# Attention and two gated MLPs on one core: three loads of weights asked for tile by tile, at other places of the pairs, one of them four pairs later

## The reference

```python
mask = q_bucket[:, :, :, None] == k_bucket[:, :, None, :]
scores = scale * np.matmul(q, k.transpose(0, 1, 3, 2))
scores = np.where(mask, scores, -1000000000.0)
attn = softmax(scores)                      # with 1e-9 added to the sum
x = np.matmul(attn, v)                      # heads side by side: (1536, 512)
h = x @ moe_w_in;   g = np.where(h > 0, h, np.exp(np.minimum(h, 0)) - 1);   x = g @ moe_w_out
h = x @ moe2_w_in;  r = np.maximum(h, 0);   g = s * r * r + b;              out = g @ moe2_w_out
```

## Time and profile before

| what | value |
|---|---|
| median of three executions | 738.39 us (738.21 to 739.23) |
| the profiled execution | 738.77 us, its span 736.9 us |
| granted TensorE clock | 0.999 |
| TensorE busy | 728.1 us, 99% of the span |
| VectorE, ScalarE, GpSimd busy | 75%, 68%, 67% |
| attention | up to about 223 us |
| loads of input weights, output weights | 96 and 32 tiles of 256 KB |

### The profile page before, as it was taken

The page is one execution under the profiler, slowest core; times in us unless marked ns, Lnnn a source line. Parts: engine busy times, 40 slices in busy tenths (PEclk is TensorE's granted clock), DMA queues, the critical chain, the costliest instruction groups (busy, mean ns, idle before and its releaser), DMA issues.

```text
span 736.9 us, 14171 instructions
## 1 busy us (share of the span) xinstructions
PE 728.1 (99%) x4617; PEld 666.1 (90%) x4617; DVE 556.4 (75%) x1185; ACT 501.6 (68%) x941; POOL 496.5 (67%) x436
## 2 busy tenths in 40 slices
PE   8999999999999999999999999999999999999998
PEld 5999999999999889988998899989998999899986
DVE  6888888888888887877666777677767776766764
ACT  7888888888885767575657666577566656474552
POOL 6678899999998687835654577677655454644340
PEclk9999999999999999999999999999999999999999
DMA  5686765665524222321112223132112211131101
GB/s 167 160 177 134 162 169 138 156 170 123 136 61 107 86 89 85 115 58 58 31 56 59 61 88 110 58 95 85 52 57 78 78 47 58 58 102 43 58 1 57
DMA packets 78287, 67.82 MB, mean 92 GB/s; under 512 B 9284, under 2 KB 66964, under 8 KB 78228
## 3 DMA queue, kind: packets, MB, share of 16 engines
q1 hardware_dynamic: 77940, 66.80, 33.6%
q10 hardware_dynamic: 288, 0.26, 0.1%
HBM read 46.23 MB, written 3.19 MB: 67 GB/s over the span
## 4 chain that ended last, share of the span: by engine, by line
PE 79%; POOL 9%; DMA 4%; issue 4%; ACT 2%; DVE 2%; SPq 0%; POOLq 0%; DVEq 0%; ACTq 0%
PE acc L939 35%; PE h_ps L919 32%; PE pt_ps L859 4%; PE pv_ps L874 2%; PE pv_ps L875 2%; PE s_ps L845 2%; PE s_ps L846 2%; POOL pt_lo L562 2%; DMA x_parts<-x_second 2%; POOL qqk L550 1%; POOL pt_hi L560 1%; DMA qqk<-qqk 1%; POOL x L578 1%; POOL x_sum L569 1%; DMA qqk<-bits 1%
## 5 line engine op out<-in xcount | busy, mean ns | idle before, releaser
L624 POOL TENSOR_TENSOR wi_lo<-w_raw,wi_hi 128x512 fp32r<-128x512 f32 x96 | 98.8, 1030 | 188.6 <-ACT wi_hi L1035 186.0
L919 PE MATMUL h_ps<-xb_hi,wi_hi 128*128 128x256 f32 x672 | 190.2, 283 | 0.5 <-DVE u_sb L1362 0.5
L919 PE MATMUL h_ps<-xb_hi,wi_lo 128*128 128x256 f32 x672 | 190.2, 283 | 0.0
L919 PE MATMUL h_ps<-xb_lo,wi_hi 128*128 128x256 f32 x672 | 190.2, 283 | 0.0
L919 PEld LDWEIGHTS h_ps<-xb_hi,wi_hi 128*128 128x128 f32 x672 | 128.8, 192 | 2.6 <-DVE u_sb L1362 0.7
L919 PEld LDWEIGHTS h_ps<-xb_lo,wi_hi 128*128 128x128 f32 x672 | 128.8, 192 | 1.8
L919 PEld LDWEIGHTS h_ps<-xb_hi,wi_lo 128*128 128x128 f32 x672 | 128.8, 192 | 0.0
L629 POOL TENSOR_TENSOR wi_lo<-wi_sum,wi_hi 128x512 fp32r<-128x512 f32 x96 | 122.6, 1298 | 1.9 <-ACT wi_hi L1035 1.9
L1157 ACT ACTIVATE r_sb<-h_sb 128x512 f32<-128x512 f32 x96 | 60.0, 625 | 76.8 <-DVE h_sb L1379 76.8
L1217 DVE TENSOR_SCALAR_CACHE_REDUCE probs<-s_ps 128x768 f32<-128x768 f32 x96 | 91.8, 957 | 10.4 <-PE s_ps L846 7.6
L939 PE MATMUL acc<-g_hi,wo_late 128*128 128x512 f32 x288 | 91.8, 390 | 0.0
(11 more groups left out here) (122 smaller groups left out, 1676.1 us busy)
## 6 DMA issues: line engine op xcount, KB each, us to landing
w_raw<-w_in_dram SPq DMA_DIRECT2D x96, 256.0 KB, 3.1
wo_raw<-w_out_dram SPq DMA_DIRECT2D x32, 256.0 KB, 2.9
raw<-qk_dram SPq DMA_DIRECT2D x15, 384.0 KB, 5.8
qqk<-kt SPq DMA_DIRECT2D x15, 384.0 KB, 4.6
raw_v<-v_dram SPq DMA_DIRECT2D x16, 192.0 KB, 4.9
x_parts<-x_second SPq DMA_DIRECT2D x16, 192.0 KB, 6.5
qqk<-qqk SPq DMA_DIRECT2D x15, 192.0 KB, 2.8
kt<-kt SPq DMA_DIRECT2D x15, 192.0 KB, 4.6
```

What stands on the lines that cost most here:

```text
L624: return nc.gpsimd.tensor_tensor(flat(lo[:, j]), w_raw[step % 2][:, cols], flat(hi[:, j]).bitcast(F32), ALU.subtract)
L919: last = mm(h_ps[bank][:, 0:Q], w[i][:, k * P:(k + 1) * P], x[j][:, k * Q:(k + 1) * Q], start=k == 0 and m == 0, stop=k == DK - 1 and m == 2)
```

## The change

The two functions that load weights get an argument that says which of the two tiles they ask for. `load_w(1)` moves from pair 1 to pair 5; `load_wo(0, 0)` and `load_wo(0, 1)` stay in pairs 2 and 4. In each of these pairs the first tile is now asked for behind `load_v(2i + 3)`, ahead of `put_inv(i, 2)`, and the second behind `move_first(i, 1)`, ahead of `put_inv(i, 3)`, the last entry of the pair. All three loads leave the place ahead of `move_second(i - 1, 1)`. Nothing else differs.

```diff
-            def load_w(step):
+            def load_w(step, tiles=range(2)):
...
-                for n in range(2):
+                for n in tiles:
                     sp.dma_start(w_raw[buf][:, n * DM:(n + 1) * DM].rearrange("p (c n) -> p c n", n=P),
                                  win_d[layer][f + n]).then_inc(w_landed[buf], 16)
-            def load_wo(layer, step):
+            def load_wo(layer, step, tiles=range(2)):
...
-                for n in range(2):
+                for n in tiles:
...
+            def load_weights(i, n):
+
+                if i == 2:
+                    load_wo(0, 0, (n,))
+                elif i == 4:
+                    load_wo(0, 1, (n,))
+                elif i == 5:
+                    load_w(1, (n,))
...
                 if i == 0:
                     load_w(0)
-                if i == 1:
-                    load_w(1)
-                if i == 2:
-                    load_wo(0, 0)
-                if i == 4:
-                    load_wo(0, 1)
                 if prev:
                     move_second(i - 1, 1)
...
                     load_v(2 * i + 3)
+                load_weights(i, 0)
                 if i == PAIRS - 2:
                     load_w(2)
                 put_inv(i, 2)
...
                 move_first(i, 1)
+                load_weights(i, 1)
                 put_inv(i, 3)
```

## The result

The change made the kernel slower: a median of 742.22 us (738.97 to 749.06, 22 executions) against 737.80 us (737.31 to 741.65, 22 executions of the kernel before beside it), a ratio of 1.006 with a 95% interval of 1.0045 to 1.0074. (A ratio here goes by all executions of both kernels, not by their medians, so a few long executions show in it and not in the median.) The forecast was 737.0 us with a range to 738.2. Two things stand out already: the kernel before is at 737.8 and not at the 738.39 us of its first three executions, and the changed kernel spreads over 10 us.

The account below looks back on a forecast made before the run. TensorE, busy 99% of the span, was taken as the bound. Stalls removed in pairs 1 and 2 and a new one at head 13, -0.64 - 0.81 + 0.10 = -1.35 us, took 738.39 to 737.0 us, range 736.6 to 738.2.

Parts of the forecast that it names:

- Both stalls go: Pairs 1 and 2: TensorE's waits for the copy of the bits vanish, worth -0.64 and -0.81 us.
- The term of -1.45 us: TensorE's losses in pairs 1 and 2 together, 0.64 and 0.81 us, taken as the ceiling of the gain.
- the carrying over to the median: Whole program: the -1.35 us from the profiled execution was applied to the three executions' median, 738.39 us, giving 737.0 us.
- nothing to speak of: Rival on pairs 1 and 2: the profiled stalls are rare in other executions; gain under 0.3 us, 738.2 us, chance 0.05.
- Pair 2 and 4, output weights: Tiles moved later in pairs 2 and 4 meet heads 7 and 11, hidden by their cover: 0 us for each.
- Pair 5, input weights: Second load_w(1) tile, directly ahead of head 13's k: priced at 1.05 us, a stall of +0.1 us.
- the rule of the two engines: get_inv in pair 5 runs on 2 of 16 DMA engines, so the tile behind it costs 1.05 rather than 2.05 us.
- What follows in pair 6 comes later by the same amount at most: Pair 6: head 14's bits and GpSimd's sums are delayed by no more than head 13's stall, put at +0.1 us.
- slower than before: Rival at head 13: one tile costs 4.1 us, so a stall of 3.2 us and 740.1 us in total, chance 0.06.

Follow-up runs that it names:

- later only: The kernel before with both tiles of load_w(1) in pair 5 instead of pair 1, at the old place ahead of move_second: 737.61 us, ratio 1.0003.
- the two splits: get_inv issued as two transfers of 64 partitions each: in the kernel before 737.41 us, ratio 0.9984; in the changed kernel 737.39 us, ratio 0.999.

## Why the prediction was wrong

*Both stalls go.* In the changed kernel none of the three profiles has a wait in pair 1 or 2. But two of three profiles of the kernel before list none there either, so that the move removes them is likely and not shown. **The size was wrong.** The term of -1.45 us was read from one execution (738.77 us); two others of the same kernel have 0.2 and 0.0 us. The signs were there: this execution was slower than two of the three executions known then, and the carrying over to the median assumed that all had the same stalls. The "nothing to speak of" rival, with a chance of 0.05, described this half of the truth; the "medians" 0.4 us apart that spoke against it were one median and one execution (738.39 and 738.77 us). The kernels without these stalls (later only, the two splits) lie at 737.4 to 737.6 us, and the fastest executions of the kernel before at 737.3.

*Pair 2 and 4, output weights.* The value of 0 held in most executions: with these loads alone at the new places the median is near that of the kernel before (ratio 1.0006, 0.9977 to 1.0035). The price was wrong here too, and the cover hid it. A tile was put at 0.85 us; k of head 7 took 5.6 to 6.8 us in the changed kernel's three profiles against 3.9 to 4.7 before, and k of head 11 5.4 and 5.5 against 3.9 to 4.2, and 8.4 in the first profile. There head 11 waited 0.78 us, so the cover for head 11 is not always enough, and "in the same way as head 7" was said without its own row.

*Pair 5, input weights.* **This is the step that failed.** The place was right (head 13, second tile) and its cover was seen as the narrowest; the price was wrong. I put a tile at 1.05 us, from a pair in which the queue had no slow transfer in it, and allowed 2.05. The prediction has `get_inv` right ahead of the second place (with `move_first` between them) and still took the low price. Measured at the place it is 9.0 - 6.2 = 2.8 us in the first profile and 3.0 and 3.3 us in the two later ones (9.1 and 9.4 against 6.1), and in pair 3 it is 9.3 - 4.6 = 4.7 us. Against a cover of 0.9 to 1.7 us that made waits of 1.6 and 1.8 us, and 3.1 where SyncE was late as well, where the prediction had 0.1. With `get_inv` split it is 3.4 - 2.5 = 0.9 us, so the 1.05 was a fair price for a tile in a queue that moves, and the wrong one for a tile behind `get_inv`. I had the rule of the two engines in hand and drew the opposite from it: that it argues for the low price. The reading that fits the runs is that `get_inv` makes late what every transfer behind it needs as well, and the tile adds its part there: with the split, k of head 13 takes 2.5 us instead of 6.1 to 6.2 without the tile, and 3.4 instead of 9.0 to 9.4 with it.

*What follows in pair 6 comes later by the same amount at most.* Wrong: after a wait TensorE's granted clock can be at its lower level for some 3 us (0.53 between 184 and 187 us after 1.75 us of wait), and 1.6 us are lost on top (17.13 - 15.38, less the 0.17 us by which that wait is longer). That term was missing altogether.

*The rival "slower than before".* It named the place and a price of 4.1 us a tile, "from a price of 2.4 to 3.2 us on". The measured 2.8 to 4.7 lies in this, and its 740.1 us is the nearest of all forecasts to 742.22. Its cause was another, what one tile does to a crowded queue, so part of this is luck. It had 0.06 because I weighed it against two stretches without `get_inv` directly ahead (pairs 2 and 6) rather than against the place itself. With executions without the stalls at 737.4 to 737.6 us and the median before at 737.8, and not 738.4, the point at which it becomes slower is lower still: a wait beyond some 0.2 to 0.4 us.

The sum with measured terms, which is bookkeeping and tests no cause, for the two later profiles: 737.44 (third profile of the kernel before) + 15.38 - 13.52 = 739.3 (measured 739.29), and 737.44 + 17.13 - 13.52 = 741.05 us (measured 740.99). What stays open: why the second tile is worse still behind `put_inv`, what happens in the long executions that no profile caught (up to 749 us in the changed kernel, 742 to 746 with `load_w(1)` at the first place, 745 and 746 with the output weights alone), and how the 2.8 to 3.3 us of the tile come about in detail: the share of each single DMA engine is in no view.

## What to carry to other kernels

A stall that one profile shows is a property of that execution until a second one shows it too: before building a sum on 0.2% of a kernel, compare the profiled execution's time with the fastest of the others. Price a moved transfer by what stands directly ahead of it at the new place, and look there for a transfer with a small slowest dimension, which here made late what stood behind it; cutting that transfer in two (here one line and two counts, 0.1 to 0.2% faster than before and a spread of 1.1 and 1.4 us instead of 7.1 on the same chip) was worth more than any order of the loads that was tried. And a short wait of TensorE can cost more than its length.

## What the runs showed of the hardware that was not expected

- Behind a transfer of 192 KB from 3 KB of memory whose slowest dimension is 2, the next one (96 KB) took 6.7 us to landing in pair 5 of the kernel before and 8.2 in the changed one; with that transfer as two of 96 KB with slowest dimension 64 it took 2.5 us in both. In the kernel before there is 1 us behind it in which the mean share of the 16 DMA engines was 0.13.
- After waits of TensorE of 1.75 and 3.08 us the granted clock went to its lower level for about 3 us (0.53 and 0.50 in the stretches shown); after one of 1.58 us, and after one of 2.06 us in another kernel, it stayed at 1.00. So the length of the wait alone doesn't say which. The executions with 1.75 and 1.58 us differ by 1.7 us of time.
- 256 KB in runs of 2048 bytes behind the same transfer still brought k of head 13 to 8.8 us, against 9.0 to 9.4 in runs of 512 bytes and 6.1 to 6.2 without a tile.
